# Sparse attention and rational MLP: every engine's order from a table, casts in separate pieces, one transfer for the constants

## The chip, the cores and the metric

The kernel runs on one core of a Trainium2 chip. The metric is the device time of one execution in microseconds (us). Five engines run their own streams of instructions, each strictly in order: TensorE (PE), VectorE (DVE), ScalarE (ACT), GpSimd (POOL) and SyncE (SP). POOL and SP only issue transfers here; POOL's transfers (queue 0) can change the type on the way, SP's (queue 1) can transpose. 16 DMA engines serve both queues.

## The reference

Attention over 8 batches of 8 heads, 576 tokens, 64 columns per head. Four heads are local (a window of 32 tokens), four are strided (tokens of the same class modulo 32). The result, 4608 tokens by 512, goes through an MLP with a rational activation.

```python
mask_local = (rel >= 0) & (rel < stride)                      # stride = 32
mask_strided = (rel >= 0) & (pos[None, :] % stride == pos[:, None] % stride)
scores = np.where(masks, scale * q @ k.T, -1e9)
attn = np.exp(scores - max); attn = attn / (sum + 1e-9)
x = (attn @ v)                                                # tokens x 512
h = x @ w_in                                                  # 512 -> 2048
P = a[0] + a[1] * h + a[2] * h2 + a[3] * h3
Q = 1.0 + np.abs(b[0]) * np.abs(h) + np.abs(b[1]) * h2
return (P / (Q + 1e-6)) @ w_out                               # 2048 -> 512
```

## The kernel before

**Stages.** For each batch b the kernel loads q, k and v, forms scores of the strided heads (stage S) and of the local heads (stage L), multiplies the probabilities with v (stages V and W), and writes x. Whenever 512 tokens of x are there, an MLP chunk can run; there are nine chunks.

**q and k.** For batches 0 and 1, `casts` brings q and k with a change of type into SBUF tiles `sg` (L564), and TensorE transposes them (`turn_qk`, L649 for local, L659 for strided heads); ACT and DVE evict them into lqT, lkT and sqkT (L668). For batches 2 to 7, `bulk` (L555) casts them from f32 to bf16 into a DRAM tensor `qk16`: four transfers per batch on POOL, and SP then loads them with DMA transposes (sqkT L619, lqT and lkT L625). V comes in eight transfers per batch on POOL (vL L579, vS L586); SP copies a shifted part of vL (L630).

**Scores and values.** TensorE lays down masks by a matmul with the identity (strided L715, local L772 and L773), adds the scores (L728, L786), DVE takes the negative row maximum (L742, L811), TensorE adds it (L749, L818) and ACT takes the exponential into pS (L755) and pL (L824, L828). The probabilities are transposed into ptS and ptL: by TensorE for batches 0 and 1 (L699), by a DMA transpose on SP for the others (L689). Sums come from a matmul with BO (L848), values from L864 (strided) and L900 (local); DVE divides (L873, L926). x goes through DRAM (`xs`, L881 to L940) and is gathered transposed into xt (L999); for the first chunks TensorE transposes it (L960, L978).

**MLP.** Per chunk: 64 matmuls with Win (L1019, each group of four is evicted by ACT into h, L1023), the activation (ACT L1040, L1054, L1059; DVE L1044 to L1074), 64 matmuls with Wout (L1091), eviction by ACT (L1099) and a store on SP (L1105). Win comes in four transfers (L596) and Wout in two (L603) on POOL.

**Constants.** The identity IDN, the masks MS and M (called M0 in the code), and BO are transferred one by one on SP (L500), the last three only after the first staged tile has landed (`late_consts`).

**What sets the order.** Every operation is recorded with a key, and the table OFF adds a number to the key of each stage. A planner (`schedule`) walks through time with estimated durations and picks on each engine the ready operation with the lowest key; `emit` writes each engine's stream in that order, with waits on semaphores. So the order on the chip is fixed, and an instruction that waits holds all that stand behind it on its engine.

Of the kernel before, what the change touches and what calls it, by code (L numbers as in the profile page):

```python
# [15 lines left out]
OFF = {  # L16
# [75 lines left out]
class Prog:  # L92
    ENG = ("pe", "act", "dve", "pool", "sp")

    def __init__(self, nc):
        self.nc = nc
        self.ops = []
        self.slow_line, self.fast_line, self.look = 6.0, 3.4, 30.0
        self.tag = None

    def op(self, eng, maker, dur, key, r=(), w=(), m=(), dma=None, occ=None, after=(), hard=(), mm=0):
# [7 lines left out]
        o.key += OFF.get(self.tag, 0.0)  # L109
# [9 lines left out]
        for d in tuple(after) + tuple(hard):  # L119
            o.deps[d] = 1  # L120
        o.hard = hard
# [82 lines left out]
    def done(self, o, fin):  # L204
        o.fin = fin
        for b in o.banks:
            b.left -= 1
            if b.left == 0:
                f = max(x.fin for x in b.ops) + 0.1
                for i in range(b.at, b.at + b.n):  # L210
                    self.blast[i] = list(b.ops)
                    self.bfree[i] = f
        for u in o.users:
            lat = (0.15 if o in u.hard else 0.035) if u.eng == o.eng and o.dma is None else 0.1
            u.ready = max(u.ready, o.fin + lat)
            u.ndep -= 1
            if u.ndep == 0:
                self.rq[u.eng].append(u)

    def schedule(self):  # L220
# [11 lines left out]
        self.rq = ready = {e: [] for e in E}  # L232
# [6 lines left out]
        for o in self.ops:  # L239
            if o.ndep == 0:  # L240
                ready[o.eng].append(o)
        left = len(self.ops)
        while left:
            best = None
            for e in E:
                q = ready[e]
                if not q:
                    continue
                t0 = free[e]
                pick = None  # L250
                block = False
                soon = None
                held = None
                for o in sorted(q, key=lambda o: (o.key, o.idx)):
                    s = max(t0, o.ready)
                    if o.bank is not None:
                        if block:
                            continue
                        at, f = self._place(o.bank.n, s)
                        if f > s + 1e-9:  # L260
                            s = f
                            if o.bank.n > 1 and o.ready <= t0 + 1e-9:
                                block = True
                    if s <= t0 + 1e-9:
                        if e == "pe":
                            st = self.reach(o, t0)[0]
                            if st > 0.2:
                                if held is None or st < held[2] - 0.3:
                                    held = (t0, o, st)
                                continue  # L270
                            if held is not None and o.key > held[1].key + self.look:
                                continue
                        pick = (t0, o)
                        break
                    if s < 1e8 and (soon is None or s < soon[0] - 1e-9):
                        soon = (s, o)
                if held is not None and pick is None:
                    pick = held[:2]
                c = pick or soon
                if c is not None and (best is None or c[0] < best[0] - 1e-9):  # L280
                    best = (c[0], e, c[1])
            if best is None:
                assert self.flow(1e6), "no bank"
# [13 lines left out]
            ready[e].remove(o)  # L297
# [113 lines left out]
def bass_strided_sparse_attn__then__act_rational_pade_kernel(nc, q, k, v, moe_w_in, moe_w_out, moe_a, moe_b, out):  # L411
# [46 lines left out]
    T_c, T_m, T_co, T_b = Tile("const"), Tile("masks"), Tile("coef"), Tile("babs")  # L458
# [18 lines left out]
    R_sg = ring("sg", 4, [72, HL, 8 * D])  # L477
# [20 lines left out]
    def const(i, dst, arr, t, after=()):  # L498
        c = nc.inline_tensor(_bf16_bits(arr), name=f"c_{i}")
        P.op("sp", lambda e, d=dst, s=c: e.dma_start(d.bitcast(u16)[:, :], s[:, :]),  # L500
             0.45, -1e6, w=[t], dma=(0.15, 2.4, 0.02), after=after)
    T_c.new()
    T_m.new()
    const(0, IDN, np.eye(128, dtype=np.float32), T_c)
# [25 lines left out]
    P.op("act", table, 1.6, -9.5e5, r=[T_w])  # L530
    TD = Banks(1)

    def tiny(e):
        r = None
        for i in range(98):
            r = e.matmul(bank(TD, 0, 2, 0, 2), warm[:, 0:2], warm[:, 0:2], start=True, stop=True, skip_group_check=True)
        return r
    P.op("pe", tiny, 3.5, -9e5, r=[T_w], w=[TD], mm=98)
# [9 lines left out]
    NPE = 2  # L548

    def casts(b, key, after=()):  # L550
        P.tag = f"c{b}"
        def bulk(s_t, h0, d_t, off, t):
            t.new()
            n = HL * S * D
# [5 lines left out]
        if b < NPE:  # L560
            for nm, s_t, h0 in (("qs", q, HL), ("ks", k, HL), ("ql", q, 0), ("kl", k, 0)):
# [5 lines left out]
                            ap=[[8 * D, 72], [S * D, HL], [1, 8 * D]])),  # L567
                    0.75, key, w=[t], dma=(1.8, 2.6, 0.098), after=after)
# [24 lines left out]
    def weights_in(i, key):  # L593
        w = Fmid // 4
# [4 lines left out]
            0.85, key, w=[T_win[i]], dma=(3.1, 2.6, 0.098))  # L599

    def weights_out(i, key, after=()):
        T_wout[i].new()
        P.op("pool", lambda e: e.dma_start(  # L603
            Wout[:, 8 * i:8 * i + 8, :],
            w_out[1024 * i:1024 * i + 1024, :].rearrange("(a p) n -> p a n", p=128)),
            0.95, key, w=[T_wout[i]], dma=(6.3, 2.6, 0.098), after=after)


    def loads(b, key, got):
# [4 lines left out]
        if b < NPE:  # L614
# [21 lines left out]
    def turn_qk(b, st, key):  # L636
# [3 lines left out]
        for nm in ("qs", "ks", "ql", "kl"):  # L640
            src = stage[b, nm]
            for pair in range(2):
                TB = Banks(1)

                def trl(e, src=src, pair=pair, TB=TB):
                    r = None
                    for j in range(8):
                        for hh in range(2):
                            r = e.transpose(  # L649
                                bankb(TB, 72 * j, 72)[64 * hh:64 * hh + 64, :],  # L650
                                src.t[0:72, 2 * pair + hh, 64 * j:64 * j + 64], IDN[0:72, 0:72],
# [3 lines left out]
                def trs(e, src=src, pair=pair, TB=TB):  # L655
                    r = None
                    for h in range(2):
                        for j in range(4):
# [511 lines left out]
```

How the kernel before makes its waits and increments, by code:

```python
            def go(eng):  # L380
                for ws, o in queues[e]:
                    for s, n in ws:
                        eng.wait_ge(s, n)
                    inst = o.maker(eng)
                    if o.dma is not None:
                        inst.then_inc(o.dst.sem, 16)
                    else:
                        inst.then_inc(sems[e], 1)
                if e == "sp":
                    for s, n in fin.items():
                        eng.wait_ge(s, n)
```

## Time and profile before

| | before |
|---|---|
| median of 3 runs | 422.89 us (420.69 to 426.59) |
| the profiled execution | 421.34 us |
| its span | 419.5 us |
| TensorE busy | 348.6 us (83%) |
| VectorE busy | 318.0 us (76%) |
| ScalarE busy | 310.6 us (74%) |
| POOL busy | 69.7 us (17%) |
| mean granted clock of TensorE | 0.938 |

The span runs from the first to the last instruction of the profiled execution; 1.84 us of its time lie outside. Busy time does not add up over the engines, since they overlap. A chain of waits follows back from the last instruction what released each piece of work; "issue" in it is time in which an engine waited for nothing that the profile shows. Landing time of a transfer is from its issue to its completion.

### The profile page before, as it was taken

The page shows a single profiled execution, that of the slowest core. Times are in us where ns is not written, and L with a number is a line of the kernel's source. Part 1 is how long each engine was busy: PE and PEld are TensorE (multiplying, and loading weights), DVE is VectorE, ACT ScalarE, POOL GpSimd, SP SyncE. Part 2 cuts the span into 40 slices and gives each one's busy share as a digit, 9 for nine tenths or more (in the row PEclk, how much of TensorE's full clock was granted, in tenths as well). Part 3 has the DMA queues.
Part 4 walks back from the last instruction along what each step waited for, and adds up shares of the span by engine and source line. Part 5 has one row for each costly group of instructions (what it writes and reads, how often), then busy time and mean ns, then how long its engine had stood idle before and what let it go on. Part 6 is the DMA issues. An engine that isn't in the chain of part 4 may idle for free.

```text
span 419.5 us, 10729 instructions
## 1 busy us (share of the span) xinstructions
PE 348.6 (83%) x4868; PEld 162.9 (39%) x4868; DVE 318.0 (76%) x256; ACT 310.6 (74%) x340; POOL 69.7 (17%) x106
## 2 busy tenths in 40 slices
PE   4364986679699889798559999899999999979596
PEld 4233443244234443344224444344444444324232
DVE  3124497892576999699918929989998997999991
ACT  2121594446368887989903999999999999999972
POOL 8483000042026008006002500000000000000000
PEclk9999998669689898999959999999999999999969
DMA  7999999569989999999999999523521300002032
GB/s 107 136 217 132 208 163 109 103 118 117 170 205 156 179 199 180 146 194 194 116 173 177 159 155 201 155 51 78 129 72 39 74 0 14 13 11 89 27 125 100
DMA packets 118029, 52.36 MB, mean 125 GB/s; under 512 B 96352, under 2 KB 111968, under 8 KB 117600
## 3 DMA queue, kind: packets, MB, share of 16 engines
q1 hardware_dynamic: 86272, 33.31, 44.3%
q0 software_dynamic: 31712, 18.37, 43.0%
q8 instruction: 38, 0.62, 0.7%
q14 instruction: 7, 0.06, 0.1%
HBM read 36.87 MB, written 20.25 MB: 136 GB/s over the span
## 4 chain that ended last, share of the span: by engine, by line
ACT 37%; PE 34%; DMA 12%; DVE 9%; issue 7%; SPq 0%; POOLq 0%
PE ps L1019 13%; PE ps L1091 11%; ACT u L1054 11%; ACT u L1059 9%; ACT h L1023 7%; ACT z L1040 6%; DMA ptS<-pS 5%; DMA ptL<-pL 3%; DMA M<-c 2%; DVE xS L873 2%; DVE u L1049 2%; PE ps L864 1%; PE ps L900 1%; DMA sg<-in_q_dram 1%; DVE h L1074 1%
## 5 line engine op out<-in xcount | busy, mean ns | idle before, releaser
L1091 PE MATMUL ps<-Wout,h 128*128 128x512 bf16 x576 | 143.7, 399 | 10.0 <-DVE h L1074 7.4
L1019 PE MATMUL ps<-xt,Win 128*128 128x512 bf16 x576 | 140.2, 390 | 7.0 <-ACT h L1023 4.3
L1023 ACT ACTIVATE h<-ps 128x512 bf16<-128x512 f32 x144 | 80.4, 627 | 19.6 <-PE ps L1019 19.3
L1091 PEld LDWEIGHTS ps<-Wout,h 128*128 128x128 bf16 x576 | 54.5, 101 | 76.8 <-DVE h L1074 9.3
L1019 PEld LDWEIGHTS ps<-xt,Win 128*128 128x128 bf16 x576 | 52.3, 100 | 73.6 <-ACT h L1023 13.3
L1054 ACT ACTIVATE u<-u,consts 128x2048 bf16<-128x2048 bf16 (+1 forms) x40 | 72.6, 1844 | 6.2 <-DVE u L1049 6.2
L1059 ACT ACTIVATE u<-u 128x2048 bf16<-128x2048 bf16 (+1 forms) x40 | 69.2, 1764 | 0.0
L1040 ACT ACTIVATE z<-h 128x2048 bf16<-128x2048 bf16 (+1 forms) x34 | 60.3, 1853 | 1.6 <-DVE h L1074 1.3
L1099 ACT ACTIVATE os<-ps 128x512 f32<-128x512 f32 x36 | 21.9, 633 | 33.8 <-PE ps L1091 32.8
L1074 DVE TENSOR_TENSOR h<-z,u 128x4096 bf16<-128x4096 bf16 (+2 forms) x21 | 41.6, 1983 | 0.6 <-ACT u L1059 0.2
L1049 DVE TENSOR_TENSOR u<-u,z 128x4096 bf16<-128x4096 bf16 (+2 forms) x21 | 41.5, 1977 | 0.3
L1070 DVE TENSOR_TENSOR z<-z,h 128x4096 bf16<-128x4096 bf16 (+2 forms) x21 | 41.6, 1981 | 0.2
L1066 DVE TENSOR_TENSOR z<-z,h 128x4096 bf16<-128x4096 bf16 (+2 forms) x21 | 41.4, 1974 | 0.1
L1047 DVE TENSOR_SCALAR u<-z,coef 128x4096 bf16<-128x4096 bf16 (+2 forms) x21 | 25.0, 1192 | 18.0 <-ACT z L1040 17.8
L555 POOL DMA_DIRECT2D qk<-in_q_dram x12 | 8.1, 678 | 151.6 <-DMA vL<-vL 151.6
L1064 DVE TENSOR_SCALAR z<-h,coef 128x4096 bf16<-128x4096 bf16 (+2 forms) x21 | 24.9, 1184 | 0.2
L579 POOL DMA_DIRECT2D vL<-in_v_dram x32 | 23.9, 758 | 4.2 <-PE ps L900 4.2
L1072 DVE TENSOR_SCALAR z<-z,coef 128x4096 bf16<-128x4096 bf16 (+2 forms) x21 | 23.7, 1128 | 0.3
L1068 DVE TENSOR_SCALAR z<-z,coef 128x4096 bf16<-128x4096 bf16 (+2 forms) x21 | 23.7, 1129 | 0.1
L900 PE MATMUL ps<-vL,ptL 64*32 64x65 bf16 x576 | 10.6, 207 | 15.2 <-DMA ptL<-pL 9.0
L586 POOL DMA_DIRECT2D vS<-in_v_dram x32 | 20.5, 651 | 4.2 <-PE ps L864 4.2
L873 DVE TENSOR_TENSOR xS<-ps,rc 128x1024 bf16<-128x1024 f32 x16 | 19.0, 1217 | 1.8 <-PE ps L864 1.6
(73 smaller groups left out, 231.5 us busy)
## 6 DMA issues: line engine op xcount, KB each, us to landing
out_dram<-os SPq DMA_DIRECT2D x36, 256.0 KB, 2.4
qk<-in_q_dram POOLq DMA_DIRECT2D x12, 288.0 KB, 7.2
qk<-in_k_dram POOLq DMA_DIRECT2D x12, 288.0 KB, 8.1
vL<-in_v_dram POOLq DMA_DIRECT2D x32, 72.0 KB, 12.4
vS<-in_v_dram POOLq DMA_DIRECT2D x32, 72.0 KB, 11.8
vL<-vL SPq DMA_DIRECT2D x16, 138.1 KB, 3.0
Win<-in_moe_w_in_dram POOLq DMA_DIRECT2D x4, 512.0 KB, 17.5
Wout<-in_moe_w_out_dram POOLq DMA_DIRECT2D x2, 1024.0 KB, 28.4
```

The costliest lines, as they stand in the source:

```text
L873: P.op("dve", lambda e, AS=AS, b2=b2: e.tensor_tensor(xb.t[:, 1024 * b2:1024 * b2 + 1024].rearrange("p (j g d) -> p j g d", j=2, d=64), ba ...
L1019: r = e.matmul(bank(ph, 0, CH), Win[:, kk, f * 128:(f + 1) * 128], xt.t[:, kk, :], start=(kk == 0), stop=(kk == NK1 - 1))
L1023: P.op("act", lambda e, f=f, ph=ph, h=h, f0=f0: e.activation(h.t[:, f - f0, :], bank(ph, 0, CH), AF.Copy), 0.6, ky, r=[ph], w=[h], occ=0.48)
L1040: P.op("act", lambda e, z=z, h=h, i=i, hp=hp: e.activation(z.t[:, hp * i:hp * i + hp, :], h.t[:, hp * i:hp * i + hp, :], AF.Abs), dact, ky ...
L1047: dv(lambda e, z=z, u=u, G_=G_: e.tensor_scalar(u.t[:, 0:G_, :], z.t[:, 0:G_, :], b1_ap, b0_ap, op0=Alu.mult, op1=Alu.add), True, 2, r=[z, ...
L1049: dv(lambda e, z=z, u=u, G_=G_: e.tensor_tensor(u.t[:, 0:G_, :], u.t[:, 0:G_, :], z.t[:, 0:G_, :], op=Alu.mult), False, 4, r=[z], m=[u])
L1054: lns.append(P.op("act", lambda e, u=u, i=i, hp=hp: e.activation(u.t[:, hp * i:hp * i + hp, :], u.t[:, hp * i:hp * i + hp, :], AF.Ln, bias ...
L1059: exs.append(P.op("act", lambda e, u=u, i=i, hp=hp: e.activation(u.t[:, hp * i:hp * i + hp, :], u.t[:, hp * i:hp * i + hp, :], AF.Exp, sca ...
L1066: dv(lambda e, z=z, h=h, G_=G_: e.tensor_tensor(z.t[:, 0:G_, :], z.t[:, 0:G_, :], h.t[:, 0:G_, :], op=Alu.mult), False, 8, r=[h], m=[z])
L1070: dv(lambda e, z=z, h=h, G_=G_: e.tensor_tensor(z.t[:, 0:G_, :], z.t[:, 0:G_, :], h.t[:, 0:G_, :], op=Alu.mult), False, 11, r=[h], m=[z])
L1074: dv(lambda e, z=z, h=h, u=u, G_=G_: e.tensor_tensor(h.t[:, 0:G_, :], z.t[:, 0:G_, :], u.t[:, 0:G_, :], op=Alu.mult), False, 14, r=[z, u], ...
L1091: r = e.matmul(bank(po, 0, Fout), h.t[:, j, m * 128:(m + 1) * 128], Wout[:, kk, :], start=(kk == 0), stop=(kk == NF - 1))
```

## The change

The table OFF is replaced by ORDER, which lists for each engine the numbers of its operations in their order; the planner picks nothing any more and only gives out PSUM banks. Besides:

- The bulk casts are written as 144 rows of 4 pieces of 256 elements, instead of rows that follow one another in memory. The transfers are 24, as before.
- All constants come in one tensor CST, 128 by 662, in one transfer at the start.
- The staged tiles `sg` have 96 partitions with 6 tokens each, instead of 72 with 8; so a transpose by TensorE takes 96 columns, and there are 12 (local) or 6 (strided) where there were 16 or 8. The eviction of a strided pair is one instruction of 576 instead of two of 288. For batches 0 and 1 sqkT keeps the tokens in their order, and the score matmuls read it with a stride (`cls`).
- Win comes in eight transfers and Wout in four.
- Warm-up matmuls: 112 instead of 98; ACT's operations all depend on the load of its table; NPE is split into three names of the same value.

Lines move down by 15 to 29: L555 is L574, L564 is L583, L715 is L733, L786 is L809, L864 is L887, L900 is L923, L1019 is L1042, L1091 is L1114.

```diff
-OFF = {
-    "G0": -45, "G1": -94.7, "G2": -151.6, "G3": -48.5, "G4": -139.1, "G5": -91.2, "G6": 69.1, "G7": 19.3,
...
+ORDER = {
+    "pe": [
+        4, 32, 30, 28, 26, 38, 86, 87, 40, 88, 89, 90, 91, 36, 92, 93, 34, 94, 102, 96, 103, 104, 98, 105, 100, 106,
...
+        given = {e: [self.ops[i] for i in ORDER[e]] for e in E}
...
-    T_win = [Tile(f"win{i}") for i in range(4)]
-    T_wout = [Tile(f"wout{i}") for i in range(2)]
-    M0 = sb("M0", [128, 512])
-    MS = sb("MS", [128, NI])
-    IDN = sb("IDN", [128, 128])
-    BO = sb("BO", [128, 4])
+    T_win = [Tile(f"win{i}") for i in range(8)]
+    T_wout = [Tile(f"wout{i}") for i in range(4)]
+    CST = sb("CST", [128, 128 + NI + 4 + 512])
+    IDN, MS, BO, M0 = CST[:, 0:128], CST[:, 128:128 + NI], CST[:, 128 + NI:132 + NI], CST[:, 132 + NI:644 + NI]
...
-    const(0, IDN, np.eye(128, dtype=np.float32), T_c)
+    cst = nc.inline_tensor(_bf16_bits(np.concatenate([np.eye(128, dtype=np.float32), ms, bo, m0], axis=1)), name="cst")
+    P.op("sp", lambda e: e.dma_start(CST.bitcast(u16)[:, :], cst[:, :]), 0.5, -1e6, w=[T_c], dma=(0.8, 2.6, 0.1))
...
-    def late_consts(first, last):
-        for i, (dst, arr) in enumerate(((MS, ms), (BO, bo), (M0, m0))):
-            const(i + 1, dst, arr, T_m, after=first)
+    def coefficients(last):
...
-                bass.AP(tensor=d_t, offset=off, ap=[[256, n // 256], [1, 256]]),
-                bass.AP(tensor=s_t.tensor, offset=s_t.offset + (b * H + h0) * S * D, ap=[[256, n // 256], [1, 256]])),
-                0.65, key, w=[t], dma=(2.1, 2.4, 0.058), after=after)
+                bass.AP(tensor=d_t, offset=off, ap=[[256, S * D // 256], [S * D, HL], [1, 256]]),
+                bass.AP(tensor=s_t.tensor, offset=s_t.offset + (b * H + h0) * S * D, ap=[[256, S * D // 256], [S * D, HL], [1, 256]])),
+                0.65, key, w=[t], dma=(1.8, 2.4, 0.065), after=after)
...
-                            ap=[[8 * D, 72], [S * D, HL], [1, 8 * D]])),
-                    0.75, key, w=[t], dma=(1.8, 2.6, 0.098), after=after)
+                            ap=[[6 * D, 96], [S * D, HL], [1, 6 * D]])),
+                    0.75, key, w=[t], dma=(1.65, 2.8, 0.075), after=after)
...
-        w = Fmid // 4
+        w = Fmid // 8
...
+        for c in range(0, Fout, 256):
+            P.op("pool", lambda e, c=c: e.dma_start(
+                Wout[:, 8 * i:8 * i + 8, c:c + 256],
+                w_out[1024 * i:1024 * i + 1024, c:c + 256].rearrange("(a p) n -> p a n", p=128)),
+                0.95, key, w=[T_wout[i]], dma=(3.2, 2.6, 0.065), after=after)
...
+        def cls(p, th, c2):
+            if pe:
+                return sqk.t[64 * p:64 * p + 64, :, :].rearrange("p x y -> p (x y)")[
+                    :, 288 * th:288 * th + 288].rearrange("p (i c) -> p c i", c=16)[:, c2, :]
+            return sqk.t[64 * p:64 * p + 64, c2, NI * th:NI * th + NI]
```

**Casts on POOL.** A row is a line, the transfer and its shape; x4 is a run of four. Before, the second Wout transfer is followed by the four casts of batch 2, then by V loads of batch 2 and the casts of batch 3:

```order
L603 DMA Wout<-in_moe_w_out_dram 128x8x512 x2
L555 DMA qk<-in_q_dram 16x9216
L555 DMA qk<-in_k_dram 16x9216
L555 DMA qk<-in_q_dram 16x9216
L555 DMA qk<-in_k_dram 16x9216
L586 DMA vS<-in_v_dram 18x4x512 x4
L579 DMA vL<-in_v_dram 32x18x64 x4
L555 DMA qk<-in_q_dram 16x9216
L555 DMA qk<-in_k_dram 16x9216
```

In the changed kernel the same place (Wout, and the casts and V loads of the batches around it) reads:

```order
L574 DMA qk<-in_k_dram 144x4x256
L598 DMA vL<-in_v_dram 32x18x64 x2
L623 DMA Wout<-in_moe_w_out_dram 128x8x256 x2
L598 DMA vL<-in_v_dram 32x18x64 x2
L605 DMA vS<-in_v_dram 18x4x512
L623 DMA Wout<-in_moe_w_out_dram 128x8x256 x2
L574 DMA qk<-in_k_dram 144x4x256
L574 DMA qk<-in_q_dram 144x4x256 x2
L605 DMA vS<-in_v_dram 18x4x512 x3
L574 DMA qk<-in_k_dram 144x4x256
```

The casts no longer stand four in a row; single ones stand between V loads and Wout, and their shape has 576 pieces instead of 16.

**TensorE in batch 1.** Before, its local scores (L786) and strided values (L864) follow one Win group:

```order
L1019 MATMUL ps<-xt,Win 128x512 x4
L786 MATMUL ps<-lkT,lqT 32x64 x16
L848 MATMUL ps<-BO,ptS 128x4 x8
L786 MATMUL ps<-lkT,lqT 32x64 x16
L864 MATMUL ps<-vS,ptS 32x64 x16
L786 MATMUL ps<-lkT,lqT 32x64 x4
L864 MATMUL ps<-vS,ptS 32x64 x80
L818 MATMUL ps<-ng,IDN 128x512 x2
```

In the changed kernel, from the same scores (L809) to the strided values (L887):

```order
L1042 MATMUL ps<-xt,Win 128x512 x4
L809 MATMUL ps<-lkT,lqT 32x64 x16
L1042 MATMUL ps<-xt,Win 128x512 x4
L809 MATMUL ps<-lkT,lqT 32x64 x20
L1042 MATMUL ps<-xt,Win 128x512 x4
L841 MATMUL ps<-ng,CST 128x512 x2
L841 MATMUL ps<-ng,CST 128x128
L1042 MATMUL ps<-xt,Win 128x512 x4
L887 MATMUL ps<-vS,ptS 32x64 x48
```

Win groups now stand between the runs of small matmuls, and the values come after the row maximum of the local heads.

**TensorE in batch 5.** Between the local heads' row maximum (L818) and their values (L900), the time in which the DMA transpose into ptL must land, before:

```order
L818 MATMUL ps<-ng,IDN 128x512 x2
L818 MATMUL ps<-ng,IDN 128x128
L1019 MATMUL ps<-xt,Win 128x512 x16
L1091 MATMUL ps<-Wout,h 128x512 x4
L1019 MATMUL ps<-xt,Win 128x512 x4
L1091 MATMUL ps<-Wout,h 128x512 x4
L1019 MATMUL ps<-xt,Win 128x512 x4
L1091 MATMUL ps<-Wout,h 128x512 x12
L900 MATMUL ps<-vL,ptL 32x65 x16
```

And the same stretch in the changed kernel:

```order
L841 MATMUL ps<-ng,CST 128x512 x2
L841 MATMUL ps<-ng,CST 128x128
L887 MATMUL ps<-vS,ptS 32x64 x16
L1114 MATMUL ps<-Wout,h 128x512 x8
L887 MATMUL ps<-vS,ptS 32x64 x16
L871 MATMUL ps<-CST,ptS 128x4 x8
L887 MATMUL ps<-vS,ptS 32x64 x64
L1042 MATMUL ps<-xt,Win 128x512 x32
L923 MATMUL ps<-vL,ptL 32x65 x16
```

44 matmuls of 512 columns stood there, now 40, with 104 small ones of the strided heads.

## Rows read from the trace of the kernel before

**Rows 1.** The page: span, busy time of the engines, the two DMA queues.

```profile
span 419.5 us, 10729 instructions
PE 348.6 (83%) x4868; PEld 162.9 (39%) x4868; DVE 318.0 (76%) x256; ACT 310.6 (74%) x340; POOL 69.7 (17%) x106
...
q1 hardware_dynamic: 86272, 33.31, 44.3%
q0 software_dynamic: 31712, 18.37, 43.0%
```

**Rows 2.** Windows: busy us (x instructions) of each engine per stretch, granted clock, DMA.

```profile
45.45:231.00 185.55, 153.40 (x2712) 70.12 (x2711) 140.19 (x111) 128.03 (x143) 36.01 (x52) 0.88 1.17 161
231.00:399.00 168.00, 154.39 (x1413) 68.25 (x1410) 152.24 (x98) 163.50 (x168) 5.86 (x9) 1.00 0.41 79
399.00:419.50 20.50, 16.80 (x64) 6.89 (x64) 10.97 (x19) 9.92 (x13) 0.00 (x0) 0.83 0.31 115
...
210.00:228.00 18.00, 13.48 (x258) 5.75 (x258) 7.08 (x8) 3.48 (x4) 0.00 (x0) 0.72 1.04 178
```

**Rows 3.** The chain that ended last: start us, us, what.

```profile
8.29 9.71 DMA M<-c
...
22.75 2.95 issue
...
34.53 4.86 issue
...
71.87 5.53 issue
...
96.18 13.02 DMA ptS<-pS
...
132.09 8.33 DMA ptS<-pS
...
201.97 12.50 DMA ptL<-pL
```

**Rows 4.** DMA landings: tile ptS, then ptL, then the page's row of vL.

```profile
DMA to landing us min/median/max: 3.0/9.3/18.5
...
DMA to landing us min/median/max: 3.2/3.9/12.5
...
vL<-in_v_dram POOLq DMA_DIRECT2D x32, 72.0 KB, 12.4
```

**Rows 5.** POOL's timeline around two sets of casts: start us, us, what, [idle before].

```profile
89.67 0.52 POOL L555 DMA_DIRECT2D qk<-in_q_dram  x1 [46.73 <-DMA vL<-vL]
...
92.55 2.64 POOL L579 DMA_DIRECT2D vL<-in_v_dram  x4
...
125.80 0.49 POOL L555 DMA_DIRECT2D qk<-in_k_dram  x1
```

**Rows 6.** Waits: engine, line, waited for, us in total, times, longest.

```profile
POOL qk L555 <- DMA vL<-vL: 151.6, 5, 46.7
...
PE ps L900 <- DMA ptL<-pL: 9.0, 1, 9.0
...
PE ps L715 <- DMA M<-c: 4.9, 1, 4.9
...
PE ps L848 <- DMA ptS<-pS: 4.4, 2, 3.3
```

**Rows 7.** TensorE's timeline around the third late transpose.

```profile
201.05 1.03 PE L1091 MATMUL ps<-Wout,h 128*128 128x512 bf16 x4
...
214.86 1.89 PE L1091 MATMUL ps<-Wout,h 128*128 128x512 bf16 x4
```

**Rows 8.** TensorE's timeline in the head.

```profile
6.37 1.14 PE L659 MATMUL ps<-IDN,sg 72*128 72x72 bf16 x16 [2.82 <-DMA sg<-in_q_dram]
...
18.64 0.69 PE L649 MATMUL ps<-IDN,sg 72*64 72x72 bf16 x16
...
20.05 0.73 PE L728 MATMUL ps<-sqkT 64*18 64x18 bf16 x64
```

More of the change, by code:

```diff
@@ L97, in __init__ @@
         self.ops = []
-        self.slow_line, self.fast_line, self.look = 6.0, 3.4, 30.0
+        self.slow_line, self.fast_line = 6.0, 3.4
         self.tag = None
+        self.first = None
     def op(self, eng, maker, dur, key, r=(), w=(), m=(), dma=None, occ=None, after=(), hard=(), mm=0):
@@ L120, in op @@
             o.deps[d] = 1
+        if eng == "act" and self.first is not None:
+            o.deps[self.first] = 1
         o.hard = hard
@@ L238, in schedule @@
         self.wbusy = {}
-        for o in self.ops:
-            if o.ndep == 0:
-                ready[o.eng].append(o)
         left = len(self.ops)
+        given = {e: [self.ops[i] for i in ORDER[e]] for e in E}
+        assert sorted(o.idx for e in E for o in given[e]) == list(range(left))
+        ptr = {e: 0 for e in E}
         while left:
@@ L245, in schedule @@
             for e in E:
-                q = ready[e]
-                if not q:
+                if ptr[e] == len(given[e]) or given[e][ptr[e]].ndep:
                     continue
[L249 to L281, printed above, removed]
+                o = given[e][ptr[e]]
+                s = max(free[e], o.ready)
+                if o.bank is not None:
+                    s = max(s, self._place(o.bank.n, s)[1])
+                if s < 1e8 and (best is None or s < best[0] - 1e-9):
+                    best = (s, e, o)
             if best is None:
-                assert self.flow(1e6), "no bank"
+                assert self.flow(1e6), "the orders wait for each other"
                 continue
@@ L476, in bass_strided_sparse_attn__then__act_rational_pade_kernel @@
     R_u = ring("u", 2, [128, G, CH])
-    R_sg = ring("sg", 4, [72, HL, 8 * D])
+    R_sg = ring("sg", 4, [96, HL, 6 * D])
     R_o = ring("os", 3, [128, Fout], f32)
@@ L529, in table @@
         return e.activation(warm[:, 2:3], warm[:, 0:1], AF.Copy)
-    P.op("act", table, 1.6, -9.5e5, r=[T_w])
+    P.first = P.op("act", table, 1.6, -9.5e5, r=[T_w])
     TD = Banks(1)
@@ L534, in tiny @@
         r = None
-        for i in range(98):
+        for i in range(112):
             r = e.matmul(bank(TD, 0, 2, 0, 2), warm[:, 0:2], warm[:, 0:2], start=True, stop=True, skip_group_check=True)
         return r
-    P.op("pe", tiny, 3.5, -9e5, r=[T_w], w=[TD], mm=98)
+    P.op("pe", tiny, 3.2, -9e5, r=[T_w], w=[TD], mm=112)
     for t in R_vL.tiles:
@@ L598, in weights_in @@
             w_in[:, i * w:(i + 1) * w].rearrange("(a p) n -> p a n", p=128)),
-            0.85, key, w=[T_win[i]], dma=(3.1, 2.6, 0.098))
+            0.85, key, w=[T_win[i]], dma=(1.6, 2.6, 0.065))
     def weights_out(i, key, after=()):
         T_wout[i].new()
[L603 to L606, printed above, removed]
+        for c in range(0, Fout, 256):
[3 more added lines that the diff above has]
+                0.95, key, w=[T_wout[i]], dma=(3.2, 2.6, 0.065), after=after)
     def loads(b, key, got):
@@ L646, in trl @@
                     r = None
-                    for j in range(8):
+                    for j in range(6):
                         for hh in range(2):
                             r = e.transpose(
-                                bankb(TB, 72 * j, 72)[64 * hh:64 * hh + 64, :],
-                                src.t[0:72, 2 * pair + hh, 64 * j:64 * j + 64], IDN[0:72, 0:72],
+                                bankb(TB, 96 * j, 96)[64 * hh:64 * hh + 64, :],
+                                src.t[:, 2 * pair + hh, 64 * j:64 * j + 64], IDN[0:96, 0:96],
                                 tile_position=(0, 64 * hh))
@@ L657, in trs, with copy @@
                     for h in range(2):
[L658 to L660 removed]
+                        for j in range(3):
+                            r = e.transpose(bankb(TB, 288 * h + 96 * j, 96),
+                                            src.t[:, 2 * pair + h, 128 * j:128 * j + 128], IDN[0:96, 0:96])
                     return r
                 if nm[1] == "l":
[L663 to L667 removed]
+                    P.op("pe", trl, 12 * 0.06, key, r=[src, T_c], w=[TB], mm=12)
+                    dst = lq if nm[0] == "q" else lk
+                    o_ = dst.t[:, S * pair:S * pair + S].rearrange("p (t j) -> p t j", j=6)
+                else:
+                    P.op("pe", trs, 6 * 0.07, key, r=[src, T_c], w=[TB], mm=6)
+                    dst = sqk
+                    c = S * pair + 2 * S * (nm[0] == "k")
+                    o_ = dst.t[:, :, :].rearrange("p x y -> p (x y)")[:, c:c + S].rearrange(
+                        "p (h t j) -> p h t j", h=2, j=3)
+                def copy(e, e_, o_, l, TB=TB):
+                    i_ = bankb(TB, 0, S)
+                    i_ = i_.rearrange("p (j t) -> p t j", j=6) if l else i_.rearrange("p (h j t) -> p h t j", h=2, j=3)
                     return e.tensor_copy(o_, i_) if e_ == "dve" else e.activation(o_, i_, AF.Copy)
@@ L849, in ssum @@
             return r
-        P.op("pe", ssum, 8 * 0.07, key, r=[ptS, T_m], w=[SB_], mm=8)
+        P.op("pe", ssum, 0.34, key, r=[ptS, T_c], w=[SB_], mm=8)
         rcS = R_rc.next()
@@ L929, in attention @@
             op=Alu.mult), 1.355, key, r=[AL, rcL], w=[xl], occ=1.27)
-        if not pe:
+        if b >= NX:
             P.op("sp", lambda e: e.dma_start(
@@ L1110, in bass_strided_sparse_attn__then__act_rational_pade_kernel @@
     vS = {0: casts(0, -100)}
-    late_consts(stage[0, "qs"].w, stage[0, "kl"].w)
+    coefficients(stage[0, "kl"].w)
     st = loads(0, -50, vS[0])
-    for i in range(4):
+    for i in range(8):
         weights_in(i, -90 + i)
@@ L1124, in bass_strided_sparse_attn__then__act_rational_pade_kernel @@
             st = loads(b + 1, key + (LK1 if b == 0 else 12), vS[b + 1])
-        xl, xb = attention(b, cur, key, b < NPE)
+        xl, xb = attention(b, cur, key)
         if b + 2 < B:
-            vS[b + 2] = casts(b + 2, key + 14, after=st["lk"].w + st["sqk"].w + st["vl"].w if b + 1 >= NPE else ())
-        if b < NPE:
+            vS[b + 2] = casts(b + 2, key + 14, after=st["lk"].w + st["sqk"].w + st["vl"].w if b + 1 >= NQ else ())
+        if b < NX:
             turn_x(b, xl, xb, key + 14)
```

69 lines of the change are left out of this document (23 added, 46 removed), and 91 rows, old and new, of tables (OFF, ORDER).

## Prediction

> **What bounds the kernel now.** The page of the profile comes first: in a span of 419.5 us TensorE is busy 348.6, VectorE 318.0, ScalarE 310.6 [rows 1]. No engine is full, so I cut the span where ScalarE (ACT) changes its habit [rows 2]. The first hidden block is evicted at 45.45 us; until then ACT works only 310.6 − 128.0 − 163.5 − 9.9 = 9.2 us. From there to 231 us, while attention and MLP are mixed, it works 128.03 of 185.55: 57.5 us idle. From 231 to 399 it works 163.50 of 168.00, so nothing is to be had there; the last 20.5 us are the 64 last Wout matmuls (16.80 us) and a store. The time lies in the first 231 us. If ACT never idled after 45.45, the end would come at 45.45 + 128.03 + 163.50 + 20.5 = 357.5: no reordering alone goes below that.
>
> The chain of waits names the idle time [rows 3]. In the head, the mask M takes 9.71 us to land. TensorE stands three times "on issue" (2.95, 4.86 and 5.53 us), waiting for nothing that the profile shows, each time in a long run of small matmuls. And three DMA transposes of probabilities take 13.02, 8.33 and 12.50 us, 33.85 together. The same operation lands in 3.0 us at best, and the median ptL in 3.9 [rows 4]. Why they are late is seen on POOL: four bulk casts go out from 89.67 on, V loads follow from 92.55 [rows 5], and the ptS issued at 96.18 lands 13 us later. The next late ptS, issued at 132.09, follows the casts that ended at 125.80 in the same way.
>
> **The change, part by part.**
>
> *Casts in pieces.* The order of POOL shows 16x9216 before, 144x4x256 now: 576 pieces of 512 B where there were 16 of 18,432 B. Nothing shows a 512 B piece by itself. Queue 0 spent 43.0% of 16 engines' 419.5 us on 31,712 packets, 91 ns each at 579 B in the mean; queue 1 44.3% on 86,272, 34.5 ns each at 386 B [rows 1]. By size, 512 B lies between: 34.5 + (512 − 386)/(579 − 386) × 56.5 = 71 ns. One old piece at queue 1's 11.2 B/ns is 1.65 us. So a transpose that shares an engine with a cast would stand behind 1.65 us at a turn now, and 0.07 us after. What it is worth is bounded by 0 (V loads, already in small pieces, hold the queue anyway) and 33.85. What was lost directly is TensorE's idle time, 9.0 and 4.4 us [rows 6]; besides, after the stall of 9.0 us, at 214.86, four Wout matmuls take 1.89 us where four took 1.03 before it [rows 7], that is the lower of the clock's two levels (1.2 GHz), and the stretch 210 to 228 was granted 0.72 [rows 2]: 2 × 0.28 × 18 = 10 us at half speed, 5 us of work lost. 9.0 + 4.4 + 5 = 18.4; I take **−17**, half of the 33.85, because V loads stay.
>
> The Trainium skill ("DMA: Bandwidth & Descriptors", Queues, rings and completion order) speaks against the full gain: an engine drains a whole packet of some 9 to 17 descriptors from one ring before it turns to the next one. By that rule the sum would be some 399, the rival of long turns below, instead of 390. No row here shows how long a turn is.
>
> *Cost of the pieces.* Per engine a cast is 36 pieces × 71 ns = 2.56 us instead of 1.65: +0.9, times 24 casts is 22 us of engine time (from −10 at 34.5 ns to +39 at 91 ns). POOL's issue price hardly moves, as V loads with 576 pieces take 2.64/4 = 0.66 us each there [rows 5]. In the forecast the 22 us lie beside computation, in the half that I don't count as gained.
>
> *One transfer for the constants, and the head.* Before, M was issued at 8.29, once the first staged tile had landed; TensorE's L715 waited 4.9 us for it last of all [rows 6]. After, the masks are with the identity in one 169 KB transfer issued at the start, ahead of all staging. One V load stands ahead of the staged tiles on POOL: 0.66 us. −4.9 + 0.7 = **−4**. If CST is slow, the first transpose (6.37 us before, [rows 8]) waits for it instead; 128 KB took 9.71 us in a crowd, so up to 5 us could be given back; it now goes out before the crowd, and I keep −4.
>
> *Staging in 96 rows.* 24 transposes fewer per batch. Sixteen take 0.69 us [rows 8], so 1 us per batch; batch 0's is in the head, batch 1's beside MLP: **−1**. Four evictions fewer on ACT and four on DVE over both batches, with the same elements: nothing. The strided reads of sqkT in the scores may cost up to a doubling, 256 × 11 ns (64 take 0.73 us, [rows 8]) = 2.9 us; the operand's bytes are the same, and I take 0. The 14 more warm-up matmuls lie in the 2.82 us in which TensorE waits for the first staged tile [rows 8].
>
> *Order on TensorE.* The 5.53 us stall sits in batch 1's strided values; ahead of it 140 small matmuls run without a 128x512 one. In the new order Win matmuls stand between the score groups there. I take that stall as gone, the two of batch 0 (no MLP work to mix in) as staying: **−5** of 13.3. The Trainium skill ("Runtime: NRT & Kernel Launch", Instruction fetch mechanics) says that fetching instructions in blocks of 256 is hidden by the issue floor; by that such a term would be 0 and the sum 395. The three issue rows show stalls of 2.95 to 5.53 us all the same, without naming fetch as their cause.
>
> The cover of the third late transpose hardly changes: 44 matmuls between L818 and L900 before, at 1.03 us per four [rows 7] 11.3 us; now 40 and 104 small ones at 11 ns, 11.4. So it can't go by order, it has to land sooner. Elsewhere the order moves much, and of 57.5 us idle some 57.5 − 33.85 − 5.53 = 18 are named neither by a DMA wait nor by that stall. I take a fifth, **−4** (0 to −12).
>
> *Weights in smaller pieces.* Wout goes behind more V loads and casts on POOL. Batch 1's attention hides it. If that cover went, the first output groups of TensorE would wait, each further transfer ahead of it costing at least POOL's 0.66 us; I take 0.
>
> **Sum.** −17 − 4 − 1 − 5 − 4 = −31. 419.5 − 31 = 388.5, and 1.84 us outside the span (421.34 − 419.5): **390 us**. The profiled run, 421.34, lies 0.4% below the median 422.89.
>
> **The rivals.**
> *Everything lands at once.* 33.85 + 13.3 + 4 + 1 = 52, nearly all of ACT's 57.5: 369. For it: a ptS can land in 3.0 [rows 4]. Against it: batch 0 has nothing to fill its issue stalls with.
> *Long turns.* An engine may serve several pieces of a cast before it turns to a transpose: one is 0.07 us, all 36 are 2.56. At the middle, 18 or 1.28 us against 1.65, 0.78 of the hold stays, 26.3 of 33.85, and the gain is 7.5: 390 + 17 − 7.5 = 399. The wait of 13.02 us after the V loads had begun speaks for it, since small pieces held the transpose up too; the median ptL of 3.9 speaks against. The Trainium skill's page "DMA: Bandwidth & Descriptors" (Queues, rings and completion order) states such turns; no run here shows one.
> *V loads are the blockers.* They follow the casts at once [rows 5] and land in 12.4 [rows 4]; no DMA gain: 390 + 17 = 407.
> *DMA engines are the bound.* Queue 0's 22 us are added while queues 0 and 1 together are 87% of 16 engines' span by packet time. Without the gain and with half of 22 on the path: 390 + 17 + 11 = 418. POOL is idle 151.6 us waiting before casts [rows 6], so there is room in time; that speaks against.
> *Casts spread over everything (slower).* The new POOL order mixes casts with V loads and sends them earlier. Then all twelve transposes of probabilities, not three, would share with casts. At a cover of about 11 us, as in batch 5, and a mean landing T, the waits are 12 × (T − 11), even with 33.85 at T = 13.8. The other terms leave 421.34 − 14 = 407; at T = 16, 60 us of waits, 26 more: 433. It decides from T = 15.8; the worst ptS so far took 18.5, the median 9.3 [rows 4].
>
> **How the numbers follow.** Forecast near 390 (378 to 402): 0.40. Long turns, 399: 0.15. All at once, 369: 0.13. V loads, 407: 0.12. These four are faster by over 2% (a run can tell about that from no change; below 414.4): 0.80. Engines full, 418: 0.12, same. Spread casts, 433: 0.08, slower. The range 366 to 414 leaves the last two out, 0.20; the cost of the pieces and of the strided reads moves the forecast inside it.
>
> **What would show it.** Right: ptS and ptL land in under 6 us in the median, and no piece of them over 8 us is in the chain; L733 (L715 before) doesn't wait for constants; the first h is evicted at about 40 us; no issue piece of 5 us in batch 1; ACT is idle some 30 us between first h and 231 instead of 57. Wrong: transposes that still take 10 us beside casts or V loads, TensorE waiting for Wout, or first h no earlier than 45.

## The result, and the profile after

The changed kernel took 401.92 us in the median of four runs (400.57 to 404.27), the kernel before 424.74 beside it: a ratio of 0.950, with a 95% interval from 0.940 to 0.960. A second set of six runs gave 0.951 (0.945 to 0.958). Some runs of every kernel come out over 1.5% longer than its fastest one; ratios leave these out, medians and ranges do not. The forecast was 390 with a range from 366 to 414, so direction and range held. The gain was 20 us in the profiled runs (421.34 to 401.23) where 31 were forecast, and it came about in another way than the prediction had it.

The page of the changed kernel, its span, busy time, the two large DMA queues and the chain by engine:

```profile
span 399.4 us, 10603 instructions
PE 336.4 (84%) x4773; PEld 161.6 (40%) x4834; DVE 317.9 (80%) x252; ACT 310.2 (78%) x336; POOL 81.2 (20%) x112
...
q1 hardware_dynamic: 85840, 33.31, 46.8%
q0 software_dynamic: 49344, 18.36, 46.2%
...
PE 36%; ACT 25%; DMA 19%; DVE 10%; issue 4%; POOL 3%; SPq 2%; ACTq 0%; POOLq 0%
```

Beside [rows 1], ACT's work is the same and the queues' share of time has grown by only 3.2 (queue 0) and 2.5 points, although queue 0 carries 17,632 packets more. The windows, cut where ACT evicts the first hidden block (41.31 us now, 45.45 before; columns as in [rows 2]):

```profile
0.00:41.31 41.31, 28.16 (x732) 19.89 (x735) 14.37 (x26) 10.06 (x16) 24.29 (x40) 1.00 1.27 158
41.31:231.00 189.69, 152.81 (x2545) 72.15 (x2579) 148.58 (x114) 139.99 (x157) 46.84 (x61) 0.90 1.33 164
231.00:380.00 149.00, 140.75 (x1442) 63.53 (x1458) 142.57 (x93) 148.13 (x147) 10.10 (x12) 1.00 0.43 83
380.00:399.40 19.40, 14.67 (x65) 6.01 (x64) 12.35 (x20) 12.01 (x18) 0.00 (x0) 0.99 0.33 122
```

ACT's idle time accounts for the 20.1 us of span. Ahead of the first hidden block it fell from 36.3 (45.45 − 9.2) to 31.25: 5.0. From there to 231 us it fell from 57.5 to 49.7: 7.8. After 231 it fell from 4.5 + 10.6 to 0.9 + 7.4: 6.8. ACT's own work is 0.4 shorter. The middle, where the forecast had ACT idle for some 30 us, is the part that fell short. The chain of waits tells why:

```profile
45.98 29.12 DMA vL<-in_v_dram
...
75.76 7.14 DMA vL<-vL
...
115.89 7.69 DMA xs<-xS
123.60 7.09 DMA xt<-xs
...
157.80 11.94 DMA sqkT<-qk
...
174.87 5.08 DMA ptS<-pS
```

The three late transposes of probabilities of [rows 3] are gone but for 5.08 us. In their place stand transfers that were not in the chain before: V of batch 1, the write and the transposed gather of x (xs, xt), and sqkT. DMA's share of the chain rose from 12% to 19%.

The 6.8 us after 231, where the prediction saw nothing to be had, were not forecast. The cut is one of time (by 231 us ACT has done 150 us of its work, before 137), but 3.2 of them lie in the last window, where the granted clock is 0.99 instead of 0.83 and the chain ends with 10 Wout matmuls (2.35 us) instead of all 64 (16.8).

### The profile page after: what moved, and what is told of

Same layout as the page of the kernel before. It is cut to its first block, busy times and chain, and to the rows that moved or that the text cites. A ratio compares the mean times of both kernels' runs of the same rounds, so it can differ in the third digit from the quotient of the medians.

```text
span 399.4 us, 10603 instructions
## 1 busy us (share of the span) xinstructions
PE 336.4 (84%) x4773; PEld 161.6 (40%) x4834; DVE 317.9 (80%) x252; ACT 310.2 (78%) x336; POOL 81.2 (20%) x112
## 4 chain that ended last, share of the span: by engine, by line
PE 36%; ACT 25%; DMA 19%; DVE 10%; issue 4%; POOL 3%; SPq 2%; ACTq 0%; POOLq 0%
PE ps L1042 14%; PE ps L1114 13%; DMA vL<-in_v_dram 7%; ACT h L1046 7%; ACT z L1063 6%; ACT u L1077 5%; ACT u L1082 5%; DMA sqkT<-qk 3%; DMA xs<-xS 2%; DMA vL<-vL 2%; DMA xt<-xs 2%; PE ps L887 2%; DMA sg<-in_k_dram 2%; DVE h L1097 2%; PE ps L923 2%
## 5 line engine op out<-in xcount | busy, mean ns | idle before, releaser
L1042 PE MATMUL ps<-xt,Win 128*128 128x512 bf16 x546 | 137.6, 396 | 21.8 <-DMA xt<-xs 7.8
L1114 PE MATMUL ps<-Wout,h 128*128 128x512 bf16 x548 | 132.9, 382 | 8.6 <-ACT h L1046 2.3
L1046 ACT ACTIVATE h<-ps 128x512 bf16<-128x512 f32 x144 | 78.8, 625 | 25.2 <-PE ps L1042 25.0
L1042 PEld LDWEIGHTS ps<-xt,Win 128*128 128x128 bf16 x576 | 53.6, 101 | 84.1 <-issue 9.5
L1114 PEld LDWEIGHTS ps<-Wout,h 128*128 128x128 bf16 x576 | 52.5, 98 | 65.1 <-DVE h L1097 2.9
L574 POOL DMA_DIRECT2D qk<-in_k_dram x12 | 11.1, 922 | 93.3 <-DMA vL<-vL 93.3
L1122 ACT ACTIVATE os<-ps 128x512 f32<-128x512 f32 x36 | 20.8, 599 | 10.3 <-PE ps L1114 6.5
L1091 DVE TENSOR_SCALAR z<-z,coef 128x4096 bf16<-128x4096 bf16 (+2 forms) x21 | 23.7, 1128 | 0.1
L605 POOL DMA_DIRECT2D vS<-in_v_dram x32 | 21.7, 681 | 6.8 <-PE ps L887 5.9
L752 PE MATMUL ps<-sqkT 64*18 64x18 bf16 x1024 | 14.5, 179 | 4.5 <-issue 4.5
```

The costliest lines, as they stand in the source:

```text
L1042: r = e.matmul(bank(ph, 0, CH), Win[:, kk, f * 128:(f + 1) * 128], xt.t[:, kk, :], start=(kk == 0), stop=(kk == NK1 - 1))
L1046: P.op("act", lambda e, f=f, ph=ph, h=h, f0=f0: e.activation(h.t[:, f - f0, :], bank(ph, 0, CH), AF.Copy), 0.6, ky, r=[ph], w=[h], occ=0.48)
L1114: r = e.matmul(bank(po, 0, Fout), h.t[:, j, m * 128:(m + 1) * 128], Wout[:, kk, :], start=(kk == 0), stop=(kk == NF - 1))
```

## The experiments

All ratios are to the kernel before, run on the same chip beside each kernel.

**Casts in long pieces in the new order (e1, e11).** In `bulk` of the changed kernel the old shape of the transfer:

```diff
-ap=[[256, S * D // 256], [S * D, HL], [1, 256]]
+ap=[[256, HL * S * D // 256], [1, 256]]
```

> The changed kernel with the casts in 16 pieces of 18,432 B again, all else (orders, constants, staging) kept. If the long pieces are what holds the transposes: ptS, ptL and the other transposes land several us later beside casts, pieces of 8 us and more for them come back into the chain, and the time is 412 to 420 us. If the order did the work and the pieces nothing: 402 us, as the changed kernel.

Four runs went from 398 to 419 us, with a median of 412.8; the spread is too wide, so it was taken again (e11_joined), with the changed kernel itself (e10_after) on the same chip.

> The kernel of e1_joined once more (the changed kernel with casts in 16 pieces of 18,432 B), for an interval: its four runs went from 398 to 419. If long pieces cost something in this order, where four casts stand alone before V loads come: 408 to 415 in the median, 6 us or more above the changed kernel, and again transposes on SP that take over 10 us to issue after casts. If that spread was chance: within 3 us of the changed kernel.

> The changed kernel itself, on the chip of the next two: 400 to 404 us.

Six runs of e11_joined: 415.5 (411.4 to 425.8), ratio 0.982 (0.975 to 0.989); the changed kernel 401.2, ratio 0.951. So in the new order short pieces are worth 0.982 − 0.951, 3.1% or 13 us, give or take some 4 by the two intervals. The landings of ptS and ptL don't show it: ptS landed in 4.5 us in the median with long pieces and in 5.0 with short ones, ptL in 4.0 with both. The timelines of POOL, SP and TensorE show one place where it went. First e11_joined, then e10_after, each with the last of four casts, the V loads behind them, SP's next gather of x, and TensorE's wait for a later one:

```profile
184.21 0.49 POOL L574 DMA_DIRECT2D qk<-in_q_dram  x1
203.86 2.00 POOL L598 DMA_DIRECT2D vL<-in_v_dram  x3 [19.16 <-PE ps L923]
...
185.03 10.46 SPq L1022 DMA_TRANSPOSE xt<-xs  x1
195.53 4.32 SPq L707 DMA_TRANSPOSE ptS<-pS  x1
...
226.48 9.87 PE L1042 MATMUL ps<-xt,Win 128*128 128x512 bf16 x32 [9.19 <-DMA xt<-xs]
```

```profile
182.11 0.77 POOL L574 DMA_DIRECT2D qk<-in_q_dram  x1
200.32 1.99 POOL L598 DMA_DIRECT2D vL<-in_v_dram  x3 [17.44 <-PE ps L923]
...
183.83 3.81 SPq L1022 DMA_TRANSPOSE xt<-xs  x1
187.68 4.50 SPq L707 DMA_TRANSPOSE ptS<-pS  x1
...
219.32 8.52 PE L1042 MATMUL ps<-xt,Win 128*128 128x512 bf16 x32 [6.40 <-DMA xt<-xs]
```

Here the four casts stand alone: V loads follow over 17 us later. Behind long pieces SP needs 10.46 us to issue one gather, behind short ones 3.81, and what stands behind it on SP comes 5 to 8 us later. TensorE stands 9.19 us instead of 6.40 for the xt that SP issues five transposes further on. That is 2.8 us, and not the whole of the 9.9 by which the two profiled spans differ (411.3 and 401.4). TensorE's waits for sqkT of batch 2 and for xt, first in e11_joined, then in e10_after, tell the stages apart:

```profile
78.06 0.66 PE L733 MATMUL ps<-CST 128*128 128x288 bf16 x2 [3.58 <-DMA sqkT<-qk]
135.23 10.30 PE L1042 MATMUL ps<-xt,Win 128*128 128x512 bf16 x36 [5.89 <-DMA xt<-xs]
```

```profile
74.12 0.66 PE L733 MATMUL ps<-CST 128*128 128x288 bf16 x2 [3.21 <-DMA sqkT<-qk]
130.76 9.30 PE L1042 MATMUL ps<-xt,Win 128*128 128x512 bf16 x36 [6.96 <-DMA xt<-xs]
```

Up to the first of these waits e11_joined loses 3.9 us, from there to the second 0.5, from there to the end of the wait for xt shown above 2.7, and behind it 2.7. The first loss lies where single casts stand between staging, V loads and Wout. So by these two traces the casts that stand alone account for under a third of the difference; no run tells what causes the rest.

**Short pieces in the old order (e2).** The same edit the other way round, in the kernel before.

> The kernel before with the casts in 576 pieces of 512 B, all else kept (same order on every engine). If the long pieces are what holds the transposes: the three waits of 13.0, 8.3 and 12.5 us shrink to under 6 each and the time falls by 10 to 17 us, to 408 to 414. If V loads hold the queue anyway: 424 us, with the three waits still there.

Ten runs: 421.3 us, ratio 0.997 (0.990 to 1.003). The gain is too small to be told from none. The late transposes in its chain:

```profile
95.83 13.96 DMA ptS<-pS
...
132.38 9.53 DMA ptS<-pS
...
168.50 13.44 DMA ptS<-pS
...
201.83 12.05 DMA ptL<-pL
```

They are as late as in [rows 3], and a fourth one has come in. In the kernel before, V loads follow at once behind each set of casts from 89.67 us on ([rows 5] has the first), and splitting the casts alone changes nothing. Its queue 0 carried 45,152 packets in 45.5% of the engines' span, against 31,712 in 43.0%: 0.455 × 419.3 − 0.430 × 419.5 is 10 us per engine for all 24 casts, 0.43 us each, where the prediction had 0.9; these are one profiled run of each.

**Less of V, less of the casts, in the old order (e5, e6).** In the kernel before, the V loads of batches 2 to 7 take 2 of 18 blocks (`NB if b < 2 else 2`); or the casts of batches 3 to 7 move a ninth, in 16 pieces of 2,048 B instead of 18,432.

> The kernel before with the V loads of batches 2 to 7 cut to a ninth (2 of 18 blocks, 2 of 18 rows; most of V is left out of the computation), all else and every order kept. If the V loads behind the casts are what holds the transposes of probabilities: the three waits of 13.0, 8.3 and 12.5 us fall below 6 each and the time to 404 to 414 us. If the casts' bytes hold them, in whatever pieces: the waits stay near 8 to 13 us and the time within 418 to 424.

> The kernel before with the casts of batches 3 to 7 cut to a ninth (their q and k are read from batch 2's place instead, so the attention of these batches is left out), V loads and every order kept. If V loads hold the transposes: the waits for ptS and ptL stay near 8 to 13 us, 416 to 423 us. If the casts hold them by their bytes: the waits fall below 6 us and the time to 404 to 414. If both do in part, each of these two runs gains some 5 to 8 us.

Both gain, and by about as much: e5 405.6 us, ratio 0.956 (0.946 to 0.965); e6 406.8 in the median of four runs (399 to 408), for which there is no interval. The kernel before took 425.4 beside them. The landing of ptS in e5_vsmall, then in e6_castsmall:

```profile
DMA to landing us min/median/max: 3.1/5.5/7.7
```

```profile
DMA to landing us min/median/max: 3.1/6.6/11.2
```

[rows 4] had 3.0/9.3/18.5. In e5_vsmall no transpose of probabilities is left among the longest pieces of the chain, in e6_castsmall one:

```profile
194.53 9.62 DMA ptL<-pL
```

Each cut takes away 19 to 20 us in the median (the expectation for "both in part" was 5 to 8 each). That is close to the 18.4 us that the prediction took as lost directly in these waits. The reading that fits is that a transpose waits for the whole burst of casts and V loads, and that cutting it from either end brings the wait under TensorE's cover; then the two gains would not add. No run makes both cuts. The shorter pieces of e6 are not its cause, if e2 is a guide, where pieces of 512 B gave nothing.

**Less of V and short pieces (e12).** The kernel of e5 with the edit of e2.

> The kernel of e5_vsmall (the kernel before, V loads of batches 2 to 7 cut to a ninth, so most of V is left out of the computation) with the casts in 576 pieces of 512 B. If the length of the pieces matters once the V loads behind the casts are out of the way: ptS lands in 3 to 5 us in the median (5.5 in e5_vsmall) and the time is 396 to 402. If it doesn't matter in this order at all: 403 to 408, as e5_vsmall.

403.0 us, ratio 0.950 (0.940 to 0.960), against 0.956 in e5: the difference lies within the intervals. ptS landed in 5.2 us in the median instead of 5.5. So in the old order the pieces' length doesn't show even with most of V gone, and what in the new order makes it worth 13 us is shown only in part.

**Pieces of 2048 B (e4).** `[[1024, S * D // 1024], [S * D, HL], [1, 1024]]` in the changed kernel.

> The changed kernel with casts in 144 pieces of 2048 B (36 rows of 4 pieces of 1024 elements). If a transpose waits for one piece of the cast at a time: pieces four times as long, still short, 402 to 405 us. If an engine serves a fixed number of pieces before it turns to the other queue (some 9 to 17): a turn is as long as before the change or longer, and the time is 410 us or more.

409.5 us in the median, 404.5 to 418.1, ratio 0.965 (0.945 to 0.985). The ratio lies between those of short pieces (0.951) and long ones (0.982), and its interval reaches both. So the runs can't tell one piece per turn from a fixed number of pieces per turn. SP's gather of x behind the four casts lies between as well, with 5.97 us to issue, and the profiled run shows larger stalls on issue (6.1 us at L752, 4.6 at L887, where the changed kernel has 2.8 and none).

**The masks at the start (e7).** In the kernel before, `after=first` is dropped and the identity goes first.

> The kernel before with the three mask transfers issued at the start of SP, no longer behind the first staged tile; on TensorE the strided mask moves ahead of one group of transposes. If the mask's landing is what delays batch 0: the wait of 4.9 us is gone, the first hidden block is evicted 3 to 5 us before 45.5, and the time falls by 3 to 5 us, to 418 to 421. If the fourth staged tile lands as late anyway, or a later wait takes it up: no change, 422 to 425.

419.4 us, ratio 0.989 (0.981 to 0.997), 4.6 us. The first hidden block, which stood at 45.45:

```profile
41.05 0.60 ACT L1023 ACTIVATE h<-ps 128x512 bf16<-128x512 f32 x1 [1.46 <-PE ps L1019]
```

So the masks alone give as much as the whole change does in the head (4.1 us, 41.31 in the changed kernel).

**V of batch 1 earlier (e3, e8).** In the changed kernel's table for POOL, the V loads of batch 2, whose first waits for batch 0's values, go behind Win, V of batch 1 and half of Wout:

```diff
-        22, 12, 11, 14, 13, 17, 18, 19, 15, 21, 16, 144, 48, 20, 53, 52, 46, 55, 143, 47, 45, 54, 61, 44, 141, 146,
-        50, 49, 60, 51, 62, 148, 147, 63, 56, 142, 145, 57, 65, 64, 58, 59, 152, 66, 67, 321, 318, 320, 329, 149,
+        22, 12, 11, 14, 13, 17, 18, 19, 15, 21, 16, 144, 48, 20, 53, 52, 46, 55, 143, 47, 45, 54, 61, 44, 141,
+        50, 49, 60, 51, 62, 63, 56, 57, 58, 59, 142, 65, 64, 146, 148, 147, 145, 152, 66, 67, 321, 318, 320, 329, 149,
```

Here 146, 148, 147 and 145 are V of batch 2, 56 to 59 V of batch 1, 64 to 67 Wout.

> The changed kernel with POOL's order changed in one place: the V loads of batch 2, of which the first waits until the local values of batch 0 are computed (14.5 us of standing), go behind the remaining Win pieces, the V loads of batch 1 and half of Wout. Those go out some 14 us earlier. If the standing of POOL is what made V of batch 1 land 29 us after its issue: no V load in the chain between 45 and 83 us, batch 1's local values some 6 to 8 us earlier, and 394 to 398 us. If the queue is full anyway, or another wait takes its place (sqkT of batch 2 on SP): 400 to 402 us.

400.9 us, ratio 0.945 (0.926 to 0.963). The interval of 8 us either way can't tell the expected gain from none. In its profiled run TensorE still waits twice, first for sqkT of batch 2, then for V, since SP's copy of batch 2's V stands ahead of batch 1's:

```profile
75.35 0.66 PE L733 MATMUL ps<-CST 128*128 128x288 bf16 x2 [6.34 <-DMA sqkT<-qk]
...
82.93 1.26 PE L923 MATMUL ps<-vL,ptL 64*32 64x65 bf16 x72 [3.50 <-DMA vL<-vL]
```

So in e8 batch 1's copies (84 and 85 in the table for SP) go ahead of 257, the transpose into sqkT:

```diff
-        0, 23, 42, 43, 24, 131, 132, 140, 259, 258, 129, 139, 130, 257, 260, 261, 161, 85, 84, 306, 452, 316, 305,
+        0, 23, 42, 43, 24, 131, 132, 140, 259, 258, 129, 139, 130, 85, 84, 257, 260, 261, 161, 306, 452, 316, 305,
```

> The kernel of e3_vfirst with one more change of place: on SP the two copies of V of batch 1 go ahead of the transpose into sqkT of batch 2 and of the copies of batch 2. In e3_vfirst they stood behind batch 2's V, which landed at 74.6 us. If this in-order wait on SP is what kept the gain of e3_vfirst away: TensorE's local values of batch 1 no longer wait for V (3.5 us), 394 to 399 us. If TensorE's wait for sqkT of batch 2 (6.3 us) sets the place anyway: 399 to 402, as e3_vfirst.

403.0 us, ratio 0.948 (0.938 to 0.957). In the profiled run, at 406.9 the longest of the four, the wait for V is gone, but TensorE stands for sqkT 3.3 us later (78.61 against 75.35), and batch 1's local values begin no sooner (84.37 against 82.93):

```profile
78.61 0.66 PE L733 MATMUL ps<-CST 128*128 128x288 bf16 x2 [6.92 <-DMA sqkT<-qk]
84.37 1.03 PE L923 MATMUL ps<-vL,ptL 64*32 64x65 bf16 x72 [1.72 <-ACT pL L851]
```

Neither version is shown to be faster than the changed kernel (0.951, 0.945 to 0.958). The same loads must be in by about 80 us in each; that their sum sets the place is a reading that fits, and no run here takes them away.

**More warm-up matmuls (e9).** 176 instead of 112 in the changed kernel.

> The changed kernel with 176 warm-up matmuls instead of 112, every order kept. In all kernels so far that share an order of TensorE, its stalls on issue come at the same instruction (in the changed one before the last 5 of a run of 80 L752, and in its variants before the last 11 of a run of 64 L887), and in the kernel before they stand 254, 382 and 128 matmuls apart. If they belong to every 128th matmul or so: with 64 more ahead, the stall in the L752 run comes 64 matmuls sooner, before the last 69, none before the last 5, and none before the last 11 of L887; the time stays within 396 to 408. If they belong to what the instruction does or waits for: they stay where they are.

402.1 us, ratio 0.953 (0.948 to 0.959). The changed kernel had this stall in the run of 80 L752, before the last 5:

```profile
49.92 0.22 PE L752 MATMUL ps<-sqkT 64*18 64x18 bf16 x5 [2.77 <-issue]
```

In e9_warm that run of 80 goes through without one. The other two places, of which the first is in batch 0:

```profile
18.63 0.19 PE L752 MATMUL ps<-sqkT 64*18 64x18 bf16 x1 [4.45 <-issue]
...
66.53 0.20 PE L887 MATMUL ps<-vS,ptS 18*32 18x64 bf16 x3 [1.77 <-issue]
```

The second is where variants of the changed kernel stall before the last 11 of the run of 64 L887, moved 64 matmuls ahead: over those 53, four L1042, four L717, and three of the run of 48 L887. So the places move with the count of matmuls, as the first of the two expectations had it; that the stall in the L752 run would stand 64 sooner did not come true, it is absent. A place is where TensorE may stall, and whether it does differs from kernel to kernel.

## Why the prediction was right and wrong

**Casts in pieces (−17): the step that failed.** Its mechanism, a transpose that stands behind one 18 KB piece at a turn, was costed as if it held wherever casts are. In the old order the edit gave −1.4 us (e2, 0.3% of 424, within its interval), although the three waits were worth about what was costed (19 us in e5 and e6); what held the transposes there was the burst of casts and V loads together. The rival of the V loads named half of it. In the new order the same edit is worth 13 us. That this is close to the term is luck: ptS and ptL, by which it was costed, land no sooner for it, the stretch with SP's gather of x behind the four casts that stand alone shows 2.7 of 9.9 us, and the rest is open. Whether an engine serves several pieces in a turn, the rival of long turns, e4 could not decide. The two parts only work together: old order with long pieces 1, with short ones 0.997; the rest of the change with long pieces 0.982, with short ones 0.951. A sum of separate terms could not hold that.

**"It can't go by order, it has to land sooner".** It did land sooner, but by order. The landing of ptL of batch 5 (12.50 us in [rows 3]) in the changed kernel, then with long pieces in the new order (e11_joined):

```profile
DMA to landing us min/median/max: 3.5/3.5/3.5
```

```profile
DMA to landing us min/median/max: 3.6/3.6/3.6
```

The median ptS also lands in 4.5 to 4.8 us there with long pieces (e11, e1), against 9.3 before. Only the cover on TensorE was counted (11.3 against 11.4 us); that POOL's new order sends the burst at another time than SP's transposes was not. In the new order ptL of batch 5 goes out at 214.68, 13 us after the last V load was issued (201.7) and 13.7 us before the next cast (228.38). So the sign that was to show the pieces at work, ptS and ptL under 6 us in the median, came true and would have done so with long pieces too.

**New waits at nothing.** Wout behind more transfers was taken at 0; V of batch 1, sqkT and xt do not occur in the sum. In the trace after, TensorE stands 4.6 us for sqkT of batch 2, 2.9 for V of batch 1, 1.3 for Wout and 7.8 for xt, 16.6 us together. A second wait for xt goes under another name:

```profile
216.55 9.32 PE L1042 MATMUL ps<-xt,Win 128*128 128x512 bf16 x31 [7.07 <-DVE z L1089]
```

In e10_after, the same kernel, the trace names the gather of xt at this place (6.40, above). These waits are more than the 11 us that the gain fell short of. How much of each reached the end was not tried; e3 and e8 moved one of them each, without a gain that their intervals show.

**Head (−4): right,** by its place and size (4.1 us in the first hidden block; e7 4.6). CST landed in 2.3 us.

**Stalls on issue (−5): right in sign, the reason was wrong.** The issue share of the chain fell from 7.1% to 4.4%, 29.8 to 17.6 us, so by 12 and not 5. The share counts every engine's, and what of it the end gained was not tried. The two stalls of batch 0 that were to stay went (2.95 and 4.86 became 0.34 and 0.94), and a new one came (2.77, L752). Of the 140 small matmuls that the prediction put ahead of the stall of 5.53, 121 stand ahead of it and 19 behind. The stalls are not tied to runs without a large matmul but to every 127th or 128th one: in the kernel before the matmuls ahead of which it stalls lie 254, 382 and 128 apart, and e9 moved one by the 64 put ahead. The Trainium skill ("Runtime: NRT & Kernel Launch", Instruction fetch mechanics) gives fetches in blocks of 256 instructions, which with a weight load for each matmul is that distance, and calls them hidden by the issue floor. The distance agrees; if the stalls are these fetches, which no run shows directly, they are not hidden: the trace before has 2.95, 4.86 and 5.53 us, the one after 2.77.

**Rest of the order (−4) and staging (−1).** The constants and all orders and staging, with long pieces, gave 1.8%, 7.8 us, of which e7's 4.6 are the masks. What is left, 3 us, answers to −5 − 4 − 1 less the new waits; the parts were not measured by themselves. The end of the kernel, which the sum leaves out, is among them: 3.2 us less of ACT's idle time in the last window. The strided reads of the scores, taken at 0, show nothing: 64 of them take 0.73 us (L752 at 13.85) as in [rows 8].

**Total.** 31 forecast and 20 measured: the 17 came to 13, by another way, and the head held. That the issue stalls and the end gave more, and that new waits for V, sqkT and xt took back the rest, is what the traces suggest; no run separates them.

## What to carry to other kernels

Before costing a change to a transfer, look at what stands next to it in the same queue, and try the change in the order in which it will run: here shorter pieces were worth nothing in the old order, where V loads follow each set of casts at once, and 3% in the new one. Count the cover on the queues as well as on the compute engine: moving the burst away from the transposes made them land sooner with pieces of either length. When a wait is removed by an order, name the load that is needed next; here it was the next wait. And choose a sign that comes true only if the mechanism does.

## What the hardware showed that was not expected

A single DMA transpose on SP held its queue's issue for 10.46 us behind four casts in 18,432 B pieces, and for 3.81 us behind the same casts in 512 B pieces. Long pieces are not the only way to this: with short ones too the transpose into lqT at 42.01 us of e10_after took 10.46 us to issue, among the loads of Win, Wout and V and a single cast. The 13,440 packets more that short casts make cost (e2) only 10 us of each DMA engine's time. TensorE's stalls on issue come at multiples of about 128 matmuls, and their size changes from run to run: before the same matmul, L864's, it was 5.53 us in the kernel before, 1.83 with short pieces (e2), and 1.08 with less of V (e5). What sets it is not shown, since two runs of one kernel, the changed one, already have 1.75 and 3.96 us before the same run of 15 L752 of a later batch.
